# Attention and two feed-forward layers in fp32 on one core: GpSimd's splitting of the second layer's weights paced by TensorE's progress, and one attention prefetch issued a weight group sooner

## The reference

```python
# q, k, v: (8, 8, 576, 64); nine chunks of 64 positions in each sequence
scores = scale * np.matmul(q_c, k_c.transpose(0, 1, 2, 4, 3))   # inside a chunk only
attn = np.exp(scores - max);  attn = attn / (sum + 1e-09);  out = np.matmul(attn, v_c)
x = out as (4608, 512)
h = x @ w_in;  x = (np.maximum(h, 0) + alpha * np.minimum(h, 0)) @ w_out      # 512 -> 2048 -> 512
h = x @ w_in2; return (h - np.tanh(h)) @ w_out2                                # 512 -> 2048 -> 512
```

## Time and profile before

| | |
|---|---|
| time of the kernel before, median of 3 runs | 1609.42 us (1609.1, 1609.42, 1614.58) |
| the profiled execution: its own time | 1612.51 us |
| the profiled execution: span | 1610.7 us |
| TensorE's granted clock over the span | 0.995 |
| busy share of TensorE, VectorE, ScalarE, GpSimd | 98%, 61%, 38%, 20% |
| GpSimd in the 40 slices of the span | busy in slices 1 to 14, idle after |
| DMA | 375.04 MB, mean 233 GB/s |

### The profile page before, as it was taken

One profiled execution on the slowest core, in us unless ns is written; L12 is line 12 of the kernel. 1 busy time (PEld: TensorE's weight loads), 2 busy tenths in 40 slices (PEclk: granted clock), 3 DMA queues, 4 the chain that ended last, 5 costly groups with the idle time before them and its releaser, 6 DMA issues.

```text
span 1610.7 us, 26636 instructions
## 1 busy us (share of the span) xinstructions
PE 1572.0 (98%) x10512; PEld 1484.8 (92%) x10512; DVE 990.4 (61%) x1371; ACT 618.9 (38%) x947; POOL 323.7 (20%) x434
## 2 busy tenths in 40 slices
PE   6999999999999999999999999999999999999999
PEld 5989998998999999999999989988988988988987
DVE  7987677867766775766674653652652662562542
ACT  5566334524533453453452331331332241241221
POOL 4964467656654200000000000000000000000000
PEclk8999999999999999999999999999999999999999
DMA  7695997698879648646736735835744744844741
GB/s 249 241 331 180 349 368 236 224 340 310 274 280 363 220 139 283 242 156 239 265 130 219 280 135 217 298 134 198 298 156 173 304 153 166 322 163 137 294 181 68
DMA packets 83146, 375.04 MB, mean 233 GB/s; under 512 B 10064, under 2 KB 23376, under 8 KB 48464
## 3 DMA queue, kind: packets, MB, share of 16 engines
q1 hardware_dynamic: 73136, 341.35, 58.9%
q0 software_dynamic: 9600, 31.46, 5.5%
q10 hardware_dynamic: 288, 0.52, 0.1%
HBM read 308.29 MB, written 65.01 MB: 232 GB/s over the span
## 4 chain that ended last, share of the span: by engine, by line
PE 85%; DVE 5%; DMA 4%; issue 3%; SPq 1%; POOL 1%; ACT 1%; ACTq 0%; DVEq 0%; POOLq 0%
PE banks L580 13%; PE banks L582 13%; PE banks L581 13%; PE banks L609 6%; PE banks L611 6%; PE banks L610 6%; PE banks L644 5%; PE banks L643 5%; PE banks L642 5%; PE a_bank L642 3%; PE a_bank L644 3%; PE a_bank L643 3%; DMA qkv<-in_chunks 2%; DMA ring<-w_split 2%; DVE go_lo L1090 1%
## 5 line engine op out<-in xcount | busy, mean ns | idle before, releaser
L580 PE MATMUL banks<-xo_hi,ring 128*128 128x384 f32 x1344 | 451.8, 336 | 5.8 <-DMA ring<-w_split 4.2
L582 PE MATMUL banks<-xo_hi,ring 128*128 128x384 f32 x1344 | 450.9, 335 | 0.0
L581 PE MATMUL banks<-xo_lo,ring 128*128 128x384 f32 x1344 | 450.8, 335 | 0.0
L1090 DVE TENSOR_TENSOR go_lo<-g_full,go_hi 128x768 fp32r<-128x768 f32 x288 | 290.9, 1017 | 226.8 <-ACT go_hi L830 226.0
L830 ACT CAST go_hi<-g_full 128x768 fp32r<-128x768 f32 x288 | 239.4, 837 | 364.5 <-PE banks L644 223.8
L609 PE MATMUL banks<-go_hi,ring 128*128 128x384 f32 x768 | 261.7, 341 | 6.9 <-DVE go_lo L1090 5.9
L580 PEld LDWEIGHTS banks<-xo_hi,ring 128*128 128x128 f32 x1344 | 253.5, 189 | 8.8 <-DMA ring<-w_split 4.8
L610 PE MATMUL banks<-go_lo,ring 128*128 128x384 f32 x768 | 257.3, 335 | 0.0
L611 PE MATMUL banks<-go_hi,ring 128*128 128x384 f32 x768 | 257.3, 335 | 0.0
L581 PEld LDWEIGHTS banks<-xo_lo,ring 128*128 128x128 f32 x1344 | 253.7, 189 | 0.4
L582 PEld LDWEIGHTS banks<-xo_hi,ring 128*128 128x128 f32 x1344 | 253.6, 189 | 0.0
(11 more groups left out here) (130 smaller groups left out, 1860.6 us busy)
## 6 DMA issues: line engine op xcount, KB each, us to landing
ring<-w_split SPq DMA_DIRECT2D x242, 1024.0 KB, 5.7
w_split<-ring SPq DMA_DIRECT2D x22, 1024.0 KB, 4.8
qkv<-in_chunks SPq DMA_DIRECT2D x60, 256.0 KB, 6.0
w_split<-made_first POOLq DMA_DIRECT2D x44, 256.0 KB, 6.3
w_split<-sums POOLq DMA_DIRECT2D x44, 256.0 KB, 5.8
y_between<-stage SPq DMA_DIRECT2D x12, 768.0 KB, 7.9
x_raw<-y_between SPq DMA_DIRECT2D x6, 1536.0 KB, 10.1
out<-x_raw SPq DMA_DIRECT2D x36, 256.0 KB, 6.5
```

The lines of the kernel that those rows point to most:

```text
L580: nc.tensor.matmul(h, hi, xo_hi[:, o, k, :], start=fresh and k == 0, stop=False, skip_group_check=not fresh)
L581: nc.tensor.matmul(h, hi, xo_lo[:, o, k, :], start=False, stop=False, skip_group_check=not fresh)
L582: last = nc.tensor.matmul(h, lo, xo_hi[:, o, k, :], start=False, stop=k == 1, skip_group_check=not fresh)
L1090: nc.vector.tensor_tensor(go_lo[:, slot, :, :], g_of(n), go_hi[:, slot, :, :], ALU.subtract).then_inc(glo_ready, 1)
```

## The change

GpSimd waits, ahead of each of the 88 blocks that it splits, for a block of TensorE's: blocks 0 to 59 for blocks 2, 6, 10, ... 46 of runs 1 to 5 (twelve in each), blocks 60 to 75 for every second block of run 5's phase B, blocks 76 to 87 for blocks 2 to 46 of run 6. Run 6's loads now each wait only for the stores that they need. And stage 2 of `load_ahead` stands behind q = 16 in place of 17.

```diff
+def made_second_order():
+
+    order = [product_at(1, i, p) for p in range(PAIRS) for i in (7, 5, 6, 3, 1, 2, 4)]
+    return order + [unit_at(1, n) - 1 + half for n in range(16) for half in range(2)]
+
+
+MADE_SECOND = made_second_order()
+
+
+def pace(k):
+
+    if k < 60:
+        return 1 + k // 12, 4 * (k % 12) + 2
+    return (SUPER - 1, 56 + 2 * (k - 60)) if k < 76 else (SUPER, 4 * (k - 76) + 2)
...
             def keep_block(j, k, src):
 
                 here = made_second if k % 2 else made_first
+                pool.wait_ge(block_done, done(*pace(k)))
                 if k >= 2:
                     pool.wait_ge(made_stored[k % 2], 16 * (k // 2))
...
-                if s == SUPER and q == 0:
+                if s == SUPER:
                     for i in range(2):
-                        sp.wait_ge(made_stored[i], 16 * BLOCKS // 2)
+                        last = max(k for k in range(i, BLOCKS, 2) if MADE_SECOND[k] // PER_GROUP <= q)
+                        sp.wait_ge(made_stored[i], 16 * (last // 2 + 1))
...
-                    if s < SUPER - 1 and q in (8, 15, 17, 18):
-                        load_ahead(s + 1, (8, 15, 17, 18).index(q))
+                    if s < SUPER - 1 and q in (8, 15, 16, 18):
+                        load_ahead(s + 1, (8, 15, 16, 18).index(q))
```

## The result

The changed kernel takes 1589.8 us in the median of four runs (1587.75 to 1594.64), the kernel before beside it 1611.39 us (1609.1 to 1614.58). The ratio is 0.9869, 95% interval 0.9837 to 0.9901: 1.3% faster, where 1598 had been forecast in a range from 1589 to 1608. The profiled execution is the slowest of the four, 1594.64 us with a span of 1592.8, so 17.9 us under the span of the profiled execution of before.

A forecast was written before the change was run, and what follows sets the result against it. TensorE, 98% busy, bounds the kernel, so only its idle time and slow stretches can be won. -11.4 - 5.6 + 2.0 + 1.4 + 0.5 = -13.1 us gave 1599.4 (profiled) or 1596.3 (median); 1598 was taken, range 1589 to 1608.

The forecast's parts named there:

- a phase A over 60 us: Sign that the prediction is wrong; phases A of runs 1 to 4 were expected between 56 and 60 us.
- the slow clock in it: Sign that the prediction is wrong: a clock under 0.97 in the phases A.
- Part 1: Phases B of runs 1 to 4: GpSimd leaves, so runs 1 to 3 look like run 4; 11.4 us less.
- Part 2: Stage 2's loads sooner in runs 1 to 4: 1.4 us each, 5.6 us less; bounds zero and 7 us.
- 79 to 80 us long: Sign that the prediction is right: length of the phases B of runs 1 to 4.
- Part 3: Phases A of runs 1 to 4, all with GpSimd's blocks: 2.0 us more; ends 6.1 less to 10.7 more.
- Part 4: Phases A of runs 5 and 6, GpSimd's traffic for the first time: 1.4 us more; ends 0 and 8.4.
- Part 5: Run 5's phase B gets 16 blocks where VectorE's cover is thin: 0.5 us more; ends 0 and 4.
- Part 6: Run 6's loads wait for single stores, GpSimd has 88 added waits: costs nothing unless a store comes late.
- Rival 1: DMA engines give the gain back in the phases A: within 0.5%, 1608 to 1611 us; chance 0.22.
- Rival 2: Stalls grow in six phases A, next group late and clock falling: 16 us slower, 1626; chance 0.06.
- Rival 3: Pacing doesn't hold, GpSimd falls behind into the phases B: 7.5 us less, about 1604; chance 0.10.

The follow-up runs named there:

- Pacing alone: The changed kernel with stage 2 of the attention's loads back behind q = 17: 1595.84 us, ratio 0.9909.
- the experiment made for it: All 88 blocks paced into the phases B, GpSimd's arithmetic cut to one column per block: 1587.47 us, against 1604.41 us with full arithmetic.
- the second profile: The changed kernel, unaltered, measured again on another chip: 1590.1 us, ratio 0.9853.
- the experiment on stage 0: The changed kernel with stage 0 of the attention's loads behind q = 11 in place of 8: 1586.92 us, ratio 0.9837.

## Why the prediction was right, and where its sizes were off

The direction and the mechanism held. The number held by little: 1589.8 us is 8 us under the forecast and 0.8 inside the range, and two of its signs of being wrong, a phase A over 60 us and the slow clock in it, appeared. In the profiled executions the parts sum to -17.6 us where the prediction has -13.1; 3.0 of the difference are in the phases B. By its parts:

- **Part 1, GpSimd out of the phases B** (11.4 us): `go_lo` at 0.95 us, the phases equal to run 4's but for part 2. Pacing alone gave 14.8 us in these phases, since it also took a part of the waits for q and k. The price of a block to VectorE, 0.58 us from the difference of two stretches, was 0.60 in the experiment made for it. The sign "79 to 80 us long" was too high: they are 78.3 and 78.4.
- **Part 2, q and k sooner** (5.6 us): here a term was too small, 1.4 us per run where it is 2.2. The step took the waits of run 4 for the time lost. TensorE's timeline of run 4 before shows what they leave out:

```profile
698.53 0.69 PE L518 MATMUL banks<-attnT,qkv 64*64 64x64 f32 x32
699.58 0.69 PE L518 MATMUL banks<-attnT,qkv 64*64 64x64 f32 x32 [0.35 <-DMA qkv<-in_chunks]
700.79 0.69 PE L494 MATMUL a_bank<-qkv 64*64 64x64 f32 x32 [0.52 <-DMA qkv<-in_chunks]
702.08 0.69 PE L494 MATMUL a_bank<-qkv 64*64 64x64 f32 x32 [0.59 <-DMA qkv<-in_chunks]
702.70 0.44 PE L609 MATMUL banks<-go_hi,ring 128*128 128x384 f32 x1
```

  and after:

```profile
682.02 1.16 PE L535 MATMUL banks<-attnT,qkv 64*64 64x64 f32 x64
683.00 1.11 PE L511 MATMUL a_bank<-qkv 64*64 64x64 f32 x64
684.04 0.45 PE L626 MATMUL banks<-go_hi,ring 128*128 128x384 f32 x1
```

  From the start of the products with v to the start of the next unit it was 702.70 - 698.53 = 4.17 us, and is 684.04 - 682.02 = 2.02: 2.15 us, the whole difference. The profile ends a matmul by a model, and the next one overlaps that end when it can follow at once: the 64 matmuls of L535 are shown with 1.16 us, though the next group starts after 0.98. So a wait that is counted from the modelled end misses a part of what each interruption costs: 1.4 counted, 2.2 lost. Against four times run 4's 80.5 us the phases B are 8.6 us shorter, over the bound of 7. Part 1 and part 2 can be told apart in another way too: with the pacing already in, the step from q = 17 to 16 gives 318.6 - 313.4 = 5.2 us in these phases, which is close to the 5.6; by the sum of both it is the pacing that brought more than the prediction gave it.
- **Part 3, phases A of runs 1 to 4** (+2.0): +1.6 in the first profile, which is near by luck. It is one phase with 5.8 us of loss, more than the 4.2 that the prediction had as the end for one, and three with 1.9 together. The loss is a scatter, not a size: in the second profile the four phases sum to 227.1 us, 3.8 under the 230.9 of before. That fits the medians having moved by 21.6 us and the profiled executions by 17.9, since the first profile is of the slowest execution; the executions without a profile do not show their phases. To take the mean of three phases that ranged from -0.2 to 4.2 was fair; to lay it on the median of the runs was not.
- **Part 4, phases A of runs 5 and 6** (+1.4): nothing. 354 and 361 GB/s with the DMA engines at 0.96 and 0.98, and no group late. Here the prediction gave the DMA engines' share too much weight. With the experiment on stage 0 it is where a large transfer stands in the queue ahead of the phase's last groups that decides; nobody moved `load_x` to try it in these two phases.
- **Part 5, run 5's phase B** (+0.5): +0.8, and 2.1 in the other execution. It happened where the cover was thinnest: ahead of unit 7 a sum (L1024) took 1.50 us for 0.95, and the two instructions of an `activate` 2.56 for 1.94. By the full exclusion that the Trainium skill states (SBUF — State Buffer, section "Who interferes with whom") the estimate for part 5 was 1.7 us, and the two profiles lie on either side of it. Single instructions do look like it: a `go_lo` of 1.98 us in the kernel with all blocks in the phases B is 1.03 over the usual. The mean per block of 0.60 us is about half of the 1.15. It is less than half of the whole arithmetic, since the 1.15 leaves out the sums of the first eight chunks: nine of 0.75 us stand in the phase of 16 blocks that gave the 0.60, which makes 1.57 us per block. So "each side loses about half the time" is more than the numbers say.
- **Part 6**: nothing, as predicted.

Rival 1, the DMA engines giving it all back, is out: the phases A of runs 1 to 4 lost 7.7 us over 56.2 in the worse execution and 2.3 in the better, before 6.1. The estimate from the 358 GB/s of the Trainium skill (DMA: Bandwidth & Descriptors, section "Where 436 GB/s comes from") asked for 2.4 us more in each loaded phase; runs 3 to 6 have 338 to 361 GB/s and lose at most 0.3. The estimate took 21 MB for a phase, and these moved 19.0 to 20.3 MB (338 GB/s over 56.5 us, 361 over 56.2), so it is the bytes that were too many. As a ceiling for short stretches the figure does not hold here: in run 1's phase A before, single slices of 1.4 us moved up to 436 GB/s. Rival 2, slower, is out by the times; run 1's 5.8 us is more than the 3.8 per phase from which that rival decides, but it is one phase of six and no second group was late behind it. Rival 3 is out too: GpSimd ran past the phases A for 2.64 us at most in the first profile and 2.94 in the second.

## What to carry to other kernels

Work of an engine that is nobody's bound still has a price by where it lies. Price it with the durations of its neighbour's instructions with and without it, then put it where the neighbour has pauses: here the same kind of arithmetic costs 2.7 to 6.4 us in a phase B and nothing that shows in a phase A. When a prefetch is a little late, ask two questions of the queue, whether it may be issued sooner and what it then stands ahead of: one step of four blocks' work gave 10 us alone (some 6 to 7 on top of the pacing), and three steps the other way for another stage gave 3 more. And a wait counted from modelled ends was too small a price here (1.4 for 2.2 us); an undisturbed instance of the same instructions, start to start, gave the right one.

## What the runs showed of the hardware

GpSimd's arithmetic on SBUF slowed VectorE by 0.60 us per block (two or three GpSimd operations of 128x256), nearly all of it in instructions that read two tensors from SBUF, while GpSimd's DMA issues and their traffic slowed them by nothing that shows (61.67 for 61.55 us of busy time).

TensorE's granted clock fell to the lower of its two levels (1.2 of 2.4 GHz, matmuls 0.32 us apart) behind waits for a weight group of 2.3 us (run 2's phase A before) and 2.7 us (run 1's after). It also fell in run 2's phase B before, behind waits for v, q and k of 0.17, 1.18 and 0.52 us within 4 us. It did not behind single waits of 1.8 us (run 3's phase A before) and 1.4 us (run 2's after), so the longest wait alone does not tell. In run 1's phase A after, the phase lost 5.8 us where the wait itself was 2.7.
